# Expert matrices loaded into attention's dead tiles, and the low halves of the second matrices subtracted on GpSimd

## The reference, cut to what matters

```
q_s = softmax(q over d); k_s = softmax(k over tokens)        # 8 batches, 8 heads, 576 tokens, 64
x   = q_s @ (k_s.T @ v)                                      # -> x: 4608 x 512

logits = x @ phi                                             # 32 slots = 8 experts x 4
slot_input = softmax(logits over tokens).T @ x               # 32 x 512
slot_out[e] = relu(slot_input[e] @ w1[e]) @ w2[e]            # w1, w2: first layer, 8 experts, 2 MB each
x = softmax(logits over slots) @ slot_out

e = argmax(x @ w_gate)                                       # second layer, one expert per token
out = gate * sigmoid(x @ w_output_gate)[e] * (relu(x @ v1[e]) @ v2[e])   # v1, v2: 8 experts, 2 MB each
```

## Time and profile before

| | us |
|---|---|
| median of 3 runs (602.79 to 605.21) | 604.61 |
| profiled execution, its own time | 606.05 |
| its span in the trace | 604.3 |
| PE busy in the span | 436.3 (72%) |
| DVE busy | 360.8 (60%) |
| ACT busy | 193.6 (32%) |
| POOL busy | 162.5 (27%) |

### The profile page before, as it was taken

The page is one execution under the profiler, slowest core; times in us unless marked ns, Lnnn a source line. Parts: engine busy times, 40 slices in busy tenths (PEclk is TensorE's granted clock), DMA queues, the critical chain, the costliest instruction groups (busy, mean ns, idle before and its releaser), DMA issues.

```text
span 604.3 us, 12802 instructions
## 1 busy us (share of the span) xinstructions
PE 436.3 (72%) x4504; PEld 252.1 (42%) x4505; DVE 360.8 (60%) x554; ACT 193.6 (32%) x310; POOL 162.5 (27%) x142
## 2 busy tenths in 40 slices
PE   0578988897376532255467638999999999999931
PEld 0556766674343322135112214554554554554420
DVE  5999999971568665456888752433433433434462
ACT  0256667674143323122322421221211211211220
POOL 2265555560000000000010031334334334334341
PEclk9999999998596756766688867999999999999955
DMA  9779999316990699985997300111111111111100
GB/s 308 250 246 376 385 387 384 117 43 238 359 336 3 231 355 371 344 308 201 348 385 291 125 6 20 38 55 55 37 55 54 38 55 54 38 56 53 36 18 1
DMA packets 44850, 106.68 MB, mean 177 GB/s; under 512 B 4560, under 2 KB 5648, under 8 KB 44816
## 3 DMA queue, kind: packets, MB, share of 16 engines
q1 hardware_dynamic: 37888, 95.42, 43.0%
q0 software_dynamic: 4816, 10.06, 5.1%
q10 hardware_dynamic: 2112, 0.71, 0.5%
HBM read 96.25 MB, written 11.88 MB: 179 GB/s over the span
## 4 chain that ended last, share of the span: by engine, by line
PE 47%; DVE 20%; issue 10%; DMA 9%; ACT 8%; POOL 3%; DVEq 0%; POOLq 0%; SPq 0%; ACTq 0%
PE banks L1423 31%; DMA kvg<-in_moe_w 5%; DMA ring<-in_moe_w 3%; DVE big L883 3%; PE banks L1410 3%; DVE top L873 3%; DVE big L740 3%; PE banks L1356 3%; ACT big L620 2%; POOL big L465 2%; PE banks L1366 2%; PE banks L1141 2%; DVE big L726 1%; DVE big L713 1%; DVE kvg L967 1%
## 5 line engine op out<-in xcount | busy, mean ns | idle before, releaser
L1423 PE MATMUL banks<-big,work 128*128 x864 | 194.0, 381 | 0.6 <-ACT work L698 0.6
L1423 PEld LDWEIGHTS banks<-big,work 128*128 128x128 f16 x864 | 83.4, 98 | 95.4 <-issue 2.8
L1082 DVE TENSOR_SCALAR work<-banks,tok,unscale 128x512 f32<-128x512 f32 x43 | 34.8, 810 | 129.6 <-PE banks L1423 127.0
L698 ACT ACTIVATE work<-banks 128x512 f16<-128x512 f32 x86 | 46.8, 595 | 188.1 <-PE banks L1410 188.1
L498 POOL DMA_INDIRECT out<-work,token_of x43 | 43.6, 1015 | 139.6 <-DVE split_ct L1064 129.5
L1074 DVE SCALAR_TENSOR_TENSOR work<-banks,work 128x512 f16<-128x512 f32 x86 | 55.1, 682 | 3.6 <-ACT work L698 3.6
L1317 PE MATMUL banks<-ring,side 128*32 128x128 f32 x384 | 20.2, 396 | 42.2 <-DMA ring<-in_moe_w 41.2
L491 POOL DMA_INDIRECT tok<-token_rows,token_of x43 | 44.2, 1027 | 21.2 <-issue 12.3
L465 POOL TENSOR_TENSOR big<-big 128x1152 f32<-128x1152 f32 x16 | 33.5, 2117 | 57.9 <-DVE big L745 57.9
L474 POOL PARTITION_ALL_REDUCE top_all<-top x8 | 2.9, 356 | 151.2 <-DVE top L873 151.2
L1141 PE MATMUL banks<-big 64*64 64x128 f32 x1152 | 38.2, 286 | 7.2 <-ACT big L526 5.9
(11 more groups left out here) (199 smaller groups left out, 568.2 us busy)
## 6 DMA issues: line engine op xcount, KB each, us to landing
ring<-in_moe_w SPq DMA_DIRECT2D x20, 2048.0 KB, 11.9
kvg<-in_moe_w SPq DMA_DIRECT2D x12, 1024.0 KB, 7.1
big<-in_k SPq DMA_DIRECT2D x8, 1152.0 KB, 6.5
big<-in_q SPq DMA_DIRECT2D x8, 1152.0 KB, 7.3
big<-in_v SPq DMA_DIRECT2D x8, 1152.0 KB, 9.2
big<-in_moe_w SPq DMA_DIRECT2D x4, 2048.0 KB, 13.8
big<-in_moe_w SPq DMA_DIRECT2D x4, 1024.0 KB, 9.3
tok<-token_rows,token_of POOLq DMA_INDIRECT x43, 2.4
```

Source lines behind the costliest of these rows:

```text
L698: act.activation(h_hi[n][:, b * 512:(b + 1) * 512], psum[2 * n + b], ACT.Relu).then_inc(h_hi_ready, 1)
L1423: return pe.matmul(psum[4 + n], h[n][:, j * P:(j + 1) * P], w_pair[:, ds(ev, 1), w, j, :].rearrange("p o n -> p (o n)"), start=j == 0 and ...
```

## The change

1. **Loads.** w1[2], w2[2], w1[3] and w2[3] go into tiles of attention as these fall free (`in_kv0` over K0 and V0, `in_kv1` over K1 and V1, `in_q` over the two Q, `in_e` over two of QE), so the tiles inside `big` are laid out anew. Experts 4 and 6 use the two last eighths of `big`, 5 and 7 the `ring`. v2 comes through three buffers in the order of experts 0, 1, 2, 3, 4, 6, 7, 5: `raw_g` (kvg), `raw_5` (the sixth eighth of `big`) and `ring_a`.
2. **The split.** ACT now makes two copies for each half of v2: the float16 high part, and the same product in float32, written over the raw half. POOL subtracts the one from the other (a `tensor_tensor`, two for each expert). DVE's low part is gone. Scales go through two columns, `scale_w`.
3. **Order.** Slots 0 and 1 run before the c chain is done, in between its steps. `slot_out` is kept once and spread four times at the end (`slot_out4`). `w_hi` stands in other places among the slots. DVE's `w_scale_of` of the last matrix stands where the low part of the last stood, behind the gate chain; ACT's `w_hi(7)` stands before the first `keep_parts`.
4. v1 comes as before through the two halves of `ring`, v1[0] into `ring_b` when slots are done, v1[1] into `ring_a` when `w_split` has reached 14.

```diff
+        ring_a, ring_b = ring[:, 0, :], ring[:, 1, :]
+        in_kv0, in_kv1, in_q, in_e = [big[:, a:a + WORDS] for a in (0, 2 * BW, 4 * BW + D, 6 * BW + D)]
+        raw_5 = big[:, 5 * WORDS:6 * WORDS]
+        raw_g = kvg[:, :]
...
+        SECOND = [(0, raw_g, raw_g_loaded, 16), (1, raw_5, raw_5_loaded, 16), (2, raw_g, raw_g_loaded, 32),
+                  (3, raw_5, raw_5_loaded, 32), (4, raw_g, raw_g_loaded, 48), (6, raw_5, raw_5_loaded, 48),
+                  (7, ring_a, raw_a_loaded, 16), (5, raw_g, raw_g_loaded, 64)]
...
@@ SP
+            sp.wait_ge(kv_done, 2 * B - 2)
+            load(in_kv0, w1, 2, kv0_loaded)
+            sp.wait_ge(q_exped, 2 * B)
+            load(in_q, w2, 2, in_q_loaded)
             sp.wait_ge(kv_done, 2 * B)
+            load(in_kv1, w1, 3, kv1_loaded)
             sp.wait_ge(y_slot_done, B)
+            load(in_e, w2, 3, in_e_loaded)
...
+            sp.wait_ge(w_split, 2)
+            load_v2(2)
+            sp.wait_ge(w_split, 4)
+            load_v2(3)
...
+            sp.wait_ge(w_split, 10)
+            load_v2(7)
+            sp.wait_ge(w_split, 14)
+            load(ring_a, v1, 1, a_loaded)
...
@@ POOL
-            def reduce_w(e):
-                pool.wait_ge(wtop_done, 2 * e + 2)
+            def split_low(k):
+                e, raw, _, _ = SECOND[k]
+                pool.wait_ge(wtop_done, 2 * k + 2)
                 pool.partition_all_reduce(top_all[:, :], top[:, :], P, bass.bass_isa.ReduceOp.max).then_inc(
                     wtop_all_done, 1)
-
-            for e in range(E):
-                reduce_w(e)
+                for u in (0, 1):
+                    pool.wait_ge(w_hi_done, 4 * k + 2 * u + 2)
+                    hi, lo = [w_pair[:, e, m, 4 * u:4 * u + 4].rearrange("p j n -> p (j n)") for m in (0, 1)]
+                    pool.tensor_tensor(lo, raw[:, u * HALF:(u + 1) * HALF], hi, ALU.subtract).then_inc(w_split, 1)
+
+            for k in range(E):
+                split_low(k)
...
@@ ACT
+            def w_hi(k, low_done=0):
...
                 for u in (0, 1):
+                    half = raw[:, u * HALF:(u + 1) * HALF]
+                    act.activation(w_pair[:, e, 0, 4 * u:4 * u + 4].rearrange("p j n -> p (j n)"), half, ACT.Copy,
+                                   scale=scale_w[:, k % 2:k % 2 + 1]).then_inc(w_hi_done, 1)
+                    act.activation(half, half, ACT.Copy, scale=scale_w[:, k % 2:k % 2 + 1]).then_inc(w_hi_done, 1)
...
@@ DVE
-            def w_low_of(e, src, parts=(0, 1)):
-                for u in parts:
-                    dve.wait_ge(w_hi_done, 2 * e + (u + 1))
...
-                    dve.scalar_tensor_tensor(lo, src[:, u * HALF:(u + 1) * HALF], scale_up[:, :], hi,
-                                             ALU.mult, ALU.subtract).then_inc(w_split, 1)
...
-            w_low_of(E - 1, v2_in)
+            w_scale_of(7)
```

More of the change, by code:

```diff
@@ L399, in _ @@
             sp.wait_ge(slot_h_done, 1)
-            load(w1_in, w1, 3, w1_loaded)
+            load(big_6, w1, 4, m6_loaded)
             sp.wait_ge(slot_o_done, 1)
[L402 to L425, removed]
+            load(big_7, w2, 4, m7_loaded)
+            sp.wait_ge(slot_h_done, 2)
@@ new lines, in _ @@
+            load(ring_b, w2, 7, b_loaded)
+            sp.wait_ge(w_split, 6)
+            load_v2(4)
+            sp.wait_ge(w_split, 8)
+            load_v2(5)
+            sp.wait_ge(slot_h_done, 8)
+            load_v2(6)
+            sp.wait_ge(slot_o_done, 8)
+            load(ring_b, v1, 0, b_loaded)
+            sp.wait_ge(w_split, 10)
+            load_v2(7)
+            sp.wait_ge(w_split, 14)
+            load(ring_a, v1, 1, a_loaded)
+            for e in range(2, E):
+                sp.wait_ge(g_parts_done, e - 1)
+                load((ring_b, ring_a)[e % 2], v1, e, (b_loaded, a_loaded)[e % 2])
@@ L626, in keep_cT, with keep_hid @@
                 act.activation(comb_T[:, 4 * n:4 * n + g, :], hview(psum[bank], g, P), ACT.Copy).then_inc(cT_copied, 1)
-            act.wait_ge(c_ready, 1)
-            act.activation(rows16[:, :, 0:NS], logit, ACT.Copy, scale=C_SCALE).then_inc(c_hi_done, 1)
-            def slots(e, split=None):
+            def keep_hid(e):
                 act.wait_ge(slot_h_done, e + 1)
@@ L650, in _ @@
             keep_cT(2, 5)
[L651 to L656, removed]
+            keep_hid(2)
+            w_hi(0)
+            keep_out(2)
+            keep_hid(3)
+            w_hi(1)
+            keep_out(3)
+            keep_hid(4)
+            keep_out(4)
+            keep_hid(5)
+            keep_out(5)
+            w_hi(2)
+            w_hi(3)
+            keep_hid(6)
+            keep_out(6)
+            keep_hid(7)
+            keep_out(7)
+            act.wait_ge(slot_out_kept, E)
+            act.wait_ge(cT_done, 3)
+            act.wait_ge(c_lo_done, 1)
+            act.activation(slot_out4, slot_out.rearrange("p c (o s) -> p c o s", o=1).to_broadcast([P, DC, 4, NS]),
+                           ACT.Copy).then_inc(slot_out_kept, 1)
+            w_hi(4)
+            w_hi(5)
+            w_hi(6)
             def g_hi(e, n):
@@ L678, in keep_parts @@
                     g_parts_kept, 1)
+            w_hi(7, 2 * E - 4)
             keep_parts(0, False)
@@ L909, in _ @@
             dve.tensor_copy(dsum4[:, 1:4, :], dsum4[:, 0:1, :].to_broadcast([P, 3, NS])).then_inc(fold_step, 1)
-            w_split_of(0, v2_0, v2_0_loaded, 16)
-            w_split_of(1, v2_1, v2_1_loaded, 16)
-            with dve.Fori(2, E - 1) as e:
-                w_split_of(e, v2_in, v2_loaded, 16 * e - 16)
+            for k in range(5):
+                w_scale_of(k)
             dve.wait_ge(gates_done, 1)
```

172 lines of the change are left out of this document (89 added, 83 removed).

## The result

The changed kernel takes 676.73 us (median of 4 runs, 674.4 to 682.3) against 604.91 us before (602.79 to 606.66): 1.120 times as long, with a 95% interval of 1.1125 to 1.128. The forecast was 676. The profiled execution has a span of 675.2 us and a time of its own of 676.91.

The account below looks back on a forecast made before the run. Between attention and the last stage the kernel waits for transfers and their request order. 176.9 + eight rounds 203.2 + memset 1.3 + gate chain 1 = 382.4, 71 us later than 311.38, giving 676 us; range 642 to 706.

Parts of the forecast that it names:

- The turns on POOL: POOL's switches between subtractions and all-reduces: 8.5 us each, between 0 and 10.7; each us counts 16 us.
- issue: POOL's idle time waiting for nothing the profile shows, in front of L492 and L497: 7 to 10 us each.
- The subtractions on POOL: POOL's float32 minus float16 over 2048 columns, two per expert: 4.0 us each, bounds 3.6 to 4.5.
- The round: POOL's work for one expert: 0.36 + 8.5 + 8.0 + 8.5 = 25.4 us, against 18.1 before.
- ACT's copies under the cover of the turn: Scale and ACT's first two copies, 4.8 us together, hidden while POOL switches to subtractions; later copies end before their subtraction.
- The first all-reduce: First all-reduce of a v2 on POOL: at 176.9 us, 4.9 later than the 172.03 before.
- The seventh round: DVE's gate chain, two-input instructions held by POOL's arithmetic: up to 8 us, 6 fit, so + 1, at most 2.
- The sum: First all-reduce of the g chain at 382.4 us, 71 later than 311.38; execution 677, median 676.
- the last stage: End of the kernel, not touched by the change; a difference over 2 us would show the forecast wrong.
- The loads: Earlier loads and three v2 buffers take the 8.20 us transfer out of each round; alone, tens of us sooner.
- Turns that cost nothing: POOL's switches near 0 after the first: round 13.2 us, time 598, faster than before; chance 0.06 for near nothing.
- The turn of 6 us: POOL's switches cheaper, about 6 us: round 20.4, time 636; chance 0.13 for 5 to 7 us.

Follow-up runs that it names:

- the first experiment: Changed kernel with the low part of each v2 back on DVE, ACT's float32 copies gone, only all-reduces on POOL, early loads kept: 601.43 us, ratio 0.9934.
- The move to POOL alone: Kernel before, its loads and order kept, with ACT's float32 copies in place and the 16 subtractions on POOL: 676.1 us, ratio 1.1148.

## Why the prediction was right, point by point

- **The turns on POOL**, 8.5 us each, bounds 0 and 10.7: right, and it is the term that carries the result. Sixteen gaps come to 51.0 + 10.05 + 60.5 + 12.78 = 134.4 us, 8.4 each, against 136. Without the 12.78, which DVE ended, fifteen are 121.6, 8.1 each. Two experiments show that it is the turns: six fewer give back 33 us, and eight pairs of them, put alone into the kernel before, cost 12 although its rounds hid most of each. That the value came so near is in part luck: 8.5 was a choice between 6 and 10.7 from one row, and each us of it is 16 us of the forecast. It had one flaw: both sides were to be alike. In front of all-reduces the gap was 8.7 in the mean of seven, in front of subtractions 7.6. And most gaps in front of L497 were put down to ACT and not, as foretold, to "issue".
- **The subtractions on POOL**, 4.0: 4.05 (L497, 4054 and 4059 ns). The Trainium skill, "GPSIMD Engine Reference", 3.1 Elementwise, states 4497 ns for a float32 `tensor_tensor` of 2048 columns; the measurement, of a form with a float16 operand and a float16 result, is a tenth below it and decides here.
- **The round**, 25.4: 25.2. Two errors meet in it: the first six rounds are 24.8 each, the seventh 28.2.
- **ACT's copies under the cover of the turn**: right; the first two end 2.6 us ahead of POOL's start (207.16 and 209.80). The experiment without all-reduces shows the cover gone: POOL then waits for ACT's copies or for the data. In the seventh round it failed, as told below.
- **The first all-reduce**, 176.9: it was at 178.17. POOL's products in attention stood 0.7 us later (119.20, before 118.51), of which the first turn of the program can explain 0.6: it took 11.31 here and 10.67 before.
- **The seventh round**, + 1 for the gate chain under lock, of at most 2: too small. The gate chain took 22.3 us (328.01 to 350.29) where the earlier trace rows had 13.6, and the all-reduce waited 12.78 us for DVE, 4 to 7 beyond a turn. DVE's timeline and the copy on ACT show two causes:

```profile
333.64 1.99 ACT L645 ACTIVATE ring<-ring,scale_w 128x2048 f32<-128x2048 f32 x1
...
336.00 0.45 DVE L977 TENSOR_REDUCE row_a<-work 128x36 f32<-128x288 f32 x1 [3.73 <-ACT work L709]
336.48 1.66 DVE L979 TENSOR_SCALAR row_a<-row_a 128x36 f32<-128x36 f32 x1
338.17 4.00 DVE L983 SCALAR_TENSOR_TENSOR row_b<-row_b,row_a 128x36 f32<-128x36 f32 x1
```

and before, for the last two:

```profile
296.49 0.18 DVE L946 TENSOR_SCALAR row_a<-row_a 128x36 f32<-128x36 f32 x1
296.70 0.20 DVE L950 SCALAR_TENSOR_TENSOR row_b<-row_b,row_a 128x36 f32<-128x36 f32 x1
```

  The gate chain's exponential (L709) stood behind ACT's four copies, two of them added by the change, and DVE was idle for 3.73 us. The prediction had looked only at the first subtraction when it called these copies hidden. Then two instructions of 36 columns ended just as POOL's subtractions did, at 338.1 and 342.1 (334.04 + 8.07 = 342.11), and took 5.3 us more than before. The first of them has one input tensor, so the hold wasn't only for instructions with two, as the prediction had it.
- **The sum**: 381.41 against 382.4 for the first all-reduce of the g chain, 70.0 us later than the earlier trace rows, with 1.3 too little at the start, 3 in the seventh round and 1.6 in front of L506, and 7.5 too much in front of the subtractions: errors of both signs that nearly cancel. From there to the last all-reduce it was 41.4 us (42.0 before), and the last stage 252.4 (250.9), within the 2 us allowed.
- **The loads**, "most of these 8 us" of a round and tens of us in all, if nothing took their place: too high for a round. Alone they gave 4 us, and 14 with the last matrix moved; there the seven rounds lost 20 us in all, 2.9 each, and the start of the first took back 5.5.
- **The rivals.** *Turns that cost nothing* was put at 598 us; the kernel without all-reduces, the nearest to it, took 602.13, though its scale no longer waited for POOL. *The turn of 6 us* is right for quiet memory in front of an all-reduce (5.94 and, with the loads held back, 5.7 to 6.0), and wrong for this kernel, in which the end of a pair releases the next load and the turn at once. Here the rule of the Trainium skill, "GPSIMD Engine Reference", 2.1 Instruction dispatch (5.95 us for a first call into freshly loaded code), agrees with the quiet turns of 5.94 and 5.93 into an all-reduce. It doesn't with the quiet ones into a subtraction (6.7 to 7.3), nor with most beside loads.

Two things stay open. What a turn does in its 6 to 10 us, no trace shows. No packet of any queue moved in two quiet ones (202.5 to 209.7, 320.9 to 326.6), and the packets of the queue that the profile calls "q8 instruction" don't follow the turns: 29 in this kernel and in the first experiment, which lacks its sixteen turns, 26 in the kernel before and in the one with turns alone. And the price of each cause in the seventh round was read from a trace, not tried by an experiment of its own.

## What to carry to other kernels

Before work is moved to an engine with slack, write down its new list and count the places where it changes from one kind of operation to another: here each turn of POOL between a `tensor_tensor` and a reduction over partitions took 6 to 11 us (once 12), and sixteen of them cost more than the transfer that the change hid. Where the mix can't be avoided, group equal operations, and don't let the event that starts a turn also start a load. And try the parts apart: the loads alone, with one scale moved, make a kernel 2.5% faster than before, inside a change that was 12% slower.

## What was not expected of the hardware

A turn is longer when a load is issued as it starts. Engines by stretch (us, five busy times with counts, granted clock, DMA share, GB/s), for the gaps of the changed kernel that were 7.98, 7.33, 10.05, 8.61 and 5.94 us long:

```profile
194.00:202.00 8.00, 0.17 (x8) 0.00 (x0) 0.00 (x0) 0.00 (x0) 0.11 (x1) 0.68 0.79 263
202.00:210.00 8.00, 0.00 (x0) 0.00 (x0) 5.17 (x7) 6.73 (x4) 0.57 (x2) 0.50 0.00 1
218.00:228.00 10.00, 4.98 (x104) 3.10 (x100) 0.00 (x0) 1.69 (x6) 0.04 (x1) 0.98 0.82 294
228.00:237.00 9.00, 3.64 (x32) 1.36 (x32) 5.17 (x7) 7.68 (x4) 0.39 (x2) 0.50 1.04 399
321.00:327.00 6.00, 0.00 (x0) 0.00 (x0) 0.00 (x0) 0.00 (x0) 0.29 (x1) 0.50 0.00 0
```

and for the first two shown of the kernel with its loads held back, 5.93 and 8.95 us:

```profile
194.00:201.00 7.00, 1.25 (x48) 0.98 (x36) 0.00 (x0) 0.00 (x0) 1.07 (x2) 0.81 0.01 2
201.00:210.00 9.00, 0.24 (x1) 0.18 (x1) 3.01 (x7) 7.84 (x5) 0.07 (x1) 0.50 0.65 233
```

Holding the loads back took five turns in front of all-reduces from 7.9 to 10.1 us down to 5.7 to 6.7. With memory quiet, the turn into subtractions (7.33) is longer than the one into an all-reduce (5.94). But the DMA share doesn't rank the turns: the first in front of subtractions took 7.46 at a share of 1.04, and the one of 10.99 in "The move to POOL alone" ran at 0.68. What decides among the turns beside loads was not tried.

And VectorE's operations on a single column are held up as well: in the kernel without all-reduces a `top_pow` of 128 x 1 took 3.42 us in the chain of waits (254.86, L901), where the same one takes 0.17 with POOL idle (285.56); it ended at 258.28, as POOL's first subtraction of that pair did (254.19 + 4.05 = 258.24).
